# A convolution and two feed-forward layers on one core: the head of the kernel rebuilt

## The reference, cut to what matters

```python
# x: (2, 4096, 192), weight_gen: (2, 4096, 8, 7), all fp32
w = exp(weight_gen - max(weight_gen, -1)); w = w / (sum(w, -1) + 1e-9)       # softmax over the 7 taps
a[s, head, :] = sum_k w[s, head, k] * x_padded[s + k, head, :]               # 8 heads of 24 columns
h = maximum(a @ w_in1, 0); b = (h * h) @ w_out1                              # 192 -> 2048 -> 192
g = b @ w_in2;             out = (g * cos(g)) @ w_out2                       # 192 -> 2048 -> 192
```

## Time and profile before

| | us |
|---|---|
| median of three runs | 1240.97 |
| lowest, highest | 1236.84, 1241.13 |
| the profiled execution | 1241.01 |
| its span | 1239.2 |
| PE busy | 1192.4 (96%) |
| DVE busy | 976.0 (79%) |
| ACT busy | 813.8 (66%) |
| POOL busy | 369.4 (30%) |

### The profile page before, as it was taken

One profiled execution on the slowest core, in us unless ns is written; L12 is line 12 of the kernel. 1 busy time (PEld: TensorE's weight loads), 2 busy tenths in 40 slices (PEclk: granted clock), 3 DMA queues, 4 the chain that ended last, 5 costly groups with the idle time before them and its releaser, 6 DMA issues.

```text
span 1239.2 us, 24972 instructions
## 1 busy us (share of the span) xinstructions
PE 1192.4 (96%) x9571; PEld 1104.4 (89%) x9571; DVE 976.0 (79%) x1497; ACT 813.8 (66%) x1471; POOL 369.4 (30%) x245
## 2 busy tenths in 40 slices
PE   2888999999999999999999999999999999999997
PEld 1555879999999999999999999999999999999986
DVE  6775768787887878788787878778787878878786
ACT  1468666676666667676666667666666666666665
POOL 3734833426133060604315070422507051000000
PEclk9887999999999999999999999999999999999999
DMA  6440101111111110011111011111111010100000
GB/s 130 108 102 20 35 12 38 21 42 19 34 26 33 27 33 12 16 37 24 33 27 33 14 27 25 22 33 27 33 24 36 9 19 2 27 2 14 1 14 14
DMA packets 112918, 37.27 MB, mean 30 GB/s; under 512 B 101536, under 2 KB 110752, under 8 KB 112800
## 3 DMA queue, kind: packets, MB, share of 16 engines
q1 hardware_dynamic: 111488, 35.19, 13.9%
q10 hardware_dynamic: 1312, 0.49, 0.2%
HBM read 23.84 MB, written 6.29 MB: 24 GB/s over the span
## 4 chain that ended last, share of the span: by engine, by line
PE 94%; DVE 3%; ACT 1%; issue 1%; DMA 1%; SPq 0%; DVEq 0%; ACTq 0%
PE y L508 46%; PE h L508 43%; PE y L537 1%; PE h L525 1%; DVE x L1037 1%; DMA xc<-in_x_dram 1%; PE h L526 0%; PE h L527 0%; PE y L538 0%; PE y L542 0%; PE y L541 0%; PE y L540 0%; DVE g_lo L1084 0%; DVE h L1047 0%; DVE gen L955 0%
## 5 line engine op out<-in xcount | busy, mean ns | idle before, releaser
L508 PE MATMUL y<-g_hi,wo 64*128 64x512 f32 x2916 | 651.7, 394 | 0.0
L508 PE MATMUL y<-g_lo,wo 64*128 64x512 f32 x1944 | 494.2, 391 | 0.0
L508 PEld LDWEIGHTS y<-g_hi,wo 64*128 64x128 f32 x2916 | 401.5, 184 | 23.4 <-DVE xa_lo L1076 2.8
L466 POOL TENSOR_TENSOR tap<-xc,gen 128x768 f32<-128x768 f32 x105 | 162.1, 1550 | 593.3 <-DVE xd_lo L1059 579.1
L508 PEld LDWEIGHTS y<-g_lo,wo 64*128 64x128 f32 x1944 | 296.1, 184 | 5.8
L863 ACT ACTIVATE turns<-turns 128x512 f32<-128x512 f32 x239 | 151.0, 632 | 190.2 <-DVE turns L1051 189.2
L1070 DVE TENSOR_TENSOR h<-h,turns 128x512 f32<-128x512 f32 x239 | 166.5, 697 | 123.3 <-ACT turns L863 122.4
L508 PE MATMUL h<-xa_hi,wa_hi 64*128 64x512 f32 x974 | 257.3, 398 | 2.5 <-DVE xd_lo L1059 1.9
L508 PE MATMUL h<-xa_hi,wa_lo 64*128 64x512 f32 x974 | 253.7, 392 | 0.0
L508 PE MATMUL h<-xa_lo,wa_hi 64*128 64x512 f32 x974 | 253.1, 392 | 0.0
L1047 DVE SCALAR_TENSOR_TENSOR h<-h,relu 128x512 f32<-128x512 f32 x256 | 178.4, 697 | 84.2 <-ACT relu L836 81.3
(11 more groups left out here) (98 smaller groups left out, 1201.6 us busy)
## 6 DMA issues: line engine op xcount, KB each, us to landing
xc<-in_x_dram SPq DMA_DIRECT2D x62, 240.0 KB
out_dram<-arena SPq DMA_DIRECT2D x64, 64.0 KB, 1.9
xt_a<-x_blocks SPq DMA_DIRECT2D x224, 16.0 KB, 1.8
arena<-in_moe_w_out_dram SPq DMA_DIRECT2D x16, 192.0 KB, 2.8
arena<-in_moe_w_in_dram SPq DMA_DIRECT2D x16, 128.0 KB, 2.4
out_dram<-arena SPq DMA_DIRECT2D x60, 32.0 KB, 1.7
xt_d<-x_blocks SPq DMA_DIRECT2D x112, 16.0 KB, 1.8
gen<-in_weight_gen_dram SPq DMA_DIRECT2D x4, 392.0 KB, 8.6
```

The source lines that it names most:

```text
L466: pool.tensor_tensor(tap[:, k % 2, :].rearrange("p (r g) -> p r g", g=GROUP), rows[k], wk, ALU.mult).then_inc(pool_step, 1)
L508: return pe.matmul(o, w[rows, :], x[rows, :], start=start, stop=stop)
```

## The change

- `piece_lo` for VectorE and GpSimd are two functions now. VectorE does pieces 0 (its input part), 2, 4 to 7, and 8, 9, 10 (`scalar_tensor_tensor` from the unscaled piece), GpSimd the output part of 0, and 1, 3 and 11 to 15. VectorE's are spread over two slots each. ScalarE scales while it writes the high part, and scales in place only for GpSimd's pieces of layer two.
- GpSimd does nothing while VectorE convolves tile 0.
- Softmax in nine parts of 4, 4, 8, 8, ... token rows; from part 2 on GpSimd subtracts the maximum (`shift`). Reduce max of parts 2 to 8 behind slots 3 to 9, the later steps where a tile needs them.
- The first slot waits for each operand in turn, not for all of them.
- From step 2 to 18 a slot is a `head_slot`: its ups and downs are halves on alternating rows. Steps 19 and 20 use the paired form without the downs of layer two.
- Tile 1 is turned behind slot 11, into y2 (tile 0: one half into y2, one into y1), which the second layer uses only from step 21. Its split is in slot 12. Tile 2 is turned at slot 6 and split at slot 11 of tile 1 (before: 10 and 15).
- The loads of the first x rows are dealt anew: quarters 0 and 1 on SyncE, 2 and 3 on ScalarE.

```diff
     def turn_at(t):
-        return (SLOTS - 3, SLOTS - 6, SLOTS // 2 - 2)[t] if t <= PEEL else TURN
+        return (SLOTS - 5, SLOTS - 10)[t] if t < PEEL else TURN
     def split_at(t):
-        return (SLOTS - 3, SLOTS - 1, SLOTS // 2 + 3)[t] if t <= PEEL else SPLIT
+        return (SLOTS - 4, SLOTS - 5)[t] if t < PEEL else SPLIT
...
-        WARM_UP = 16
-        HI_AFTER = {(0, 0): (2,), (0, 2): (3,), (0, 4): (4,), (0, 6): (5,), (0, 8): (6,), (0, 10): (7,),
-                    (0, 11): (8,), (0, 12): (9,), (0, 13): (10,), (0, 14): (11,),
-                    (1, 0): (12,), (1, 1): (13,), (1, 2): (14,), (1, 3): (15,)}
-        LO_AFTER = {(0, 1): (2,), (0, 3): (3,), (0, 5): (4,), (0, 7): (5,), (0, 9): (6,), (0, 11): (7,)}
-        POOL_PIECES = range(PL, PIECES)
-        PARTS = [0, 2 * JJ, 6 * JJ, 11 * JJ, OWN]
-        SOFTMAX_AFTER = {(0, 2): [(1, 0)], (0, 3): [(1, 1)], (0, 6): [(1, 2), (1, 3)],
-                         (0, 8): [(2, 0)], (0, 10): [(2, 1)], (0, 12): [(3, 0)], (0, 13): [(3, 1)],
-                         (1, 0): [(2, 2), (2, 3)], (1, 1): [(3, 2), (3, 3)]}
-        EXPS_AFTER = {(0, 4): (1,), (0, 15): (2, 3)}
+        WARM_UP = 12
+        HI_AT = {4: 2, 5: 4, 6: 6, 7: 8, 8: 9, 9: 11, 10: 13, 11: 14, 12: 16, 13: 18, 14: 22, 15: 25}
+        for pc, n in HI_AT.items():
+            for op in range(3):
+                HI_AFTER.setdefault(n + op * (n > SLOTS), []).append((pc, op))
+        LO_AT = {2: 2, 4: 4, 5: 6, 6: 8, 7: 10, 8: 12, 9: 14, 10: 18}
+        POOL_LO = (3, 11, 12, 13, 14, 15)
+        for pc, n in LO_AT.items():
+            LO_AFTER.setdefault(n, []).extend([(pc, 0), (pc, 1)])
+            LO_AFTER.setdefault(n + 1, []).append((pc, 2))
+        PARTS = [0] + [JJ * t for t in range(1, TILES + 1) if t == 1 or t % 2 == 0]
+        LOADS = [0, 2, 5, len(PARTS) - 1]
+        SOFTMAX_AFTER = {0: [(1, 2), (1, 3)]}
+        SOFTMAX_AFTER.update({n: [(n - 1, 0)] for n in range(3, 10)})
+        SOFTMAX_AFTER.update({12: [(2, 2)], 13: [(2, 3)], 29: [(3, 2)], 30: [(3, 3)]})
+        SOFTMAX_AFTER.update({2 * SLOTS + 6 + k: [(4 + k // 2, 2 + k % 2)] for k in range(10)})
+        EXPS_AFTER = {n: n - 9 for n in range(11, 18)}
+        SIN_AFTER = 17
...
+            pool.wait_ge(piece_ready[0], 2)
+            for op in range(2):
+                piece_lo(1, op)
+            piece_lo(0, 2)
+            piece_lo(1, 2)
+            for op in range(3):
+                piece_lo(3, op)
+            scale(1)
+            pool.wait_ge(gen_scaled, 2)
             pool.wait_ge(x_loaded, FIRST_X + NEXT_X)
             convolve(1)
+            for part in range(2, len(PARTS) - 1):
+                shift(part)
+            scale(2)
+            pool.wait_ge(gen_scaled, 3)
             pool.wait_ge(x_loaded, FIRST_X + NEXT_X * 2)
             convolve(2)
+            for pc in POOL_LO[1:]:
+                for op in range(3):
+                    piece_lo(pc, op)
...
+            def head_slot(t, i, par, o, down):
+                n = SLOTS * t + i
+                fresh = i == D1 and t > 0
+                ups_of_slot(t, i, n, n - LAG)
+                if fresh:
+                    for k in range(3):
+                        up_a(o, 0, i, par, TOP, k, start=k == 0)
+                downs_of_slot(n, n - LAG)
+                y1_free(t, i, y1_summed)
...
+                for k in range(2):
+                    if not fresh:
+                        up_a(o, 0, i, par, TOP, k, start=k == 0)
+                    last = down_d(down, BOTTOM, k, start=k == 0)
+                last.then_inc(y1_d_left, 1)
+                if not fresh:
+                    up_a(o, 0, i, par, TOP, 2)
+                y1_free(t, i, y1_read)
...
+                for k in range(3):
+                    last = down_a(down, BOTTOM, k, start=k == 0)
+                    last_up = up_d(o, 0, i, par, k)
...
+                down_d(down, TOP, 0)
+                down_d(down, TOP, 1, stop=True).then_inc(y1_d_done, 1)
+                pe.wait_ge(y1_a_left, n - D1 + 1)
+                down_a(down, TOP, 0)
+                pe.wait_ge(h1_left, n - D1 + 1)
+                up_a(o, 0, i, par, BOTTOM, 0)
+                down_a(down, TOP, 1)
+                up_a(o, 0, i, par, BOTTOM, 1)
+                down_a(down, TOP, 2, stop=True).then_inc(down1_done, 1)
+                up_a(o, 0, i, par, BOTTOM, 2, stop=True).then_inc(up1_done, 1)
+                if (t, i) == (0, turn_at(0)):
+                    pe.wait_ge(x1_ready, 1)
+                    pe.wait_ge(x1_split, 2)
+                    for part in range(2):
+                        turn_x1(1, part)
...
+                last = act.activation(hi, w, ACT.Copy, scale=by)
+                if l and pc in POOL_LO:
+                    last = act.activation(w, w, ACT.Copy, scale=by)
```

More of the change, by code:

```diff
@@ L498, in _ @@
             for t in range(3, TILES):
+                if t % 2 == 0:
+                    scale(t // 2 + 1)
+                    pool.wait_ge(gen_scaled, t // 2 + 2)
                 pool.wait_ge(x_loaded, FIRST_X + NEXT_X * t)
@@ L555, in down_d, with turn_x1 @@
                             stop=stop and f == SLOTS - 1)
-            def turn_x1(i, part):
+            def turn_x1(t, part):
                 for jj in range(JJ):
                     at = jj * DM + part * DA
-                    for side, bank in enumerate(turn_banks(i)):
+                    for side in range(2):
                         rows = slice(side * DD, (side + 1) * DD)
-                        o = h[:, bank, part * TOK // 2:(part + 1) * TOK // 2].rearrange("p (q j n) -> p j q n", j=JJ, n=BLOCK)
+                        o = turn_banks(t, part)[:, side, part * TOK // 2:(part + 1) * TOK // 2].rearrange(
+                            "p (q j n) -> p j q n", j=JJ, n=BLOCK)
                         last = pe.transpose(o[:, jj], x1[rows, at:at + P], ident[rows, rows])
[L565 to L572, removed]
+                last.then_inc(x1_turned, 1)
             def ups_of_slot(t, i, n, m):
@@ L949, in softmax @@
                 if op == 0:
-                    dve.wait_ge(gen_loaded[min(part, 1)], 16 * QUARTERS)
+                    dve.wait_ge(gen_loaded[sum(part >= a for a in LOADS[1:])], 16 * QUARTERS)
                     dve.tensor_reduce(stat_view(part), gen_view(part), axis=AX.X,
@@ L1010, in tail_chunk, with piece_lo, low @@
                     turn_y2_d(TILES - 2)
+            def piece_lo(pc, op):
+                l, q = divmod(pc, PL)
+                r = pc % RING
+                cols = slice(q * PIECE, (q + 1) * PIECE)
+                fs = slice(q * PF, (q + 1) * PF)
+                rows = slice(l * DD, (l + 1) * DD)
+                by = [INV_2PI, 2.0 * math.pi] if l else [1.0, 1.0]
+                dve.wait_ge(piece_hi[pc], op + 1)
+                if op:
+                    dve.wait_ge(piece_ready[pc], op)
+                def low(o, w, hi, by):
+                    if l == 0:
+                        return dve.tensor_tensor(o, w, hi, ALU.subtract)
+                    return dve.scalar_tensor_tensor(o, w, by, hi, ALU.mult, ALU.subtract)
+                if op == 0:
+                    last = low(wa_lo[l][:, cols], stage_a[:, r, :], wa_hi[l][:, cols], by[0])
+                elif op == 1:
+                    last = low(wd_lo[rows, cols], stage_d[rows, r, :], wd_hi[rows, cols], by[0])
+                else:
+                    low(wo[l][:, fs, DM:2 * P], stage_o[:, r, :, DA:DM], wo[l][:, fs, DA:DM], by[1])
+                    last = low(wo[l][:, fs, 2 * P:2 * DM], stage_o[:, r, :, 0:DA], wo[l][:, fs, 0:DA], by[1])
+                last.then_inc(piece_ready[pc], 1)
             def convolve_first():
@@ L1091, in _ @@
             dve.memset(x1[:, JJ * DM:], 0.0).then_inc(pad_zeroed, 1)
-            for op in range(4):
+            for part in range(2):
+                for op in range(2):
+                    softmax(part, op)
+            for op in range(2, 4):
                 softmax(0, op)
```

323 lines of the change are left out of this document (157 added, 166 removed).

## The result

The changed kernel takes 1219.4 us (median of four runs, 1218.3 to 1220.5), the kernel before beside it 1239.9; the ratio is 0.984, 95% interval 0.982 to 0.986. 1218.0 us was forecast. The profiled execution took 1220.16 us against 1241.01: 20.9 us less.

A forecast was written before the change was run, and what follows sets the result against it. Only the head could move, with VectorE, made to wait beside GpSimd, setting much of its pace. Slot 22 starting 19.3 us earlier and 3.7 us from slot 32 took 1241.0 to 1218.0 us; range 1203 to 1231.

The forecast's parts named there:

- the walk: The prediction's slot-by-slot timing of the head from the start: slot 10 at 66.5 us, slot 18 at 91, slot 22 at 109.
- the three signs that I had named for being wrong: VectorE waiting for the convolution in slot 22, TensorE waiting for a piece's low part, or half clock past 40 us.
- First convolution: VectorE's start of the head: with GpSimd idle its 13 instructions take 12.0 us, ending at 23.7 us, 2.8 us earlier.
- Head slot of 2.6 us: TensorE from slot 2: halves on alternating rows take 2.6 us at full clock against 2.96, about 4.8 at half clock.
- the rival of 1222 us: TensorE's head slots: weight loads between same-row halves are exposed, costing 4.6 us in all; chance 0.04.
- VectorE bound, slots 3 to 9: VectorE, stretched beside GpSimd until 58.5 us, sets the time at 3.2 to 5.4 us a slot; slot 10 at 66.5.
- The price of these waits: Rival in the head: with piece work never waiting for GpSimd, slots 3 to 9 cost 2.9, not 4.3 us; chance 0.18.
- a case that stays low throughout: TensorE's clock: half-row matmuls don't bring it up, slots 2 to 18 take 4.8 us each, total 1256 us; chance 0.06.
- Slots 10 to 17: Late head: slot 10 starts at 66.5 us and slot 18 at 91, against 69.93 and 101.99 before.
- Slots 18 to 21: End of the head: slot 18 at 91 us, slot 22 at 109 instead of 128.27, three slots in 13.5 us.
- Slot 32: The stall waiting for tile 2's split goes, as tile 2 is turned and split earlier: 3.7 us gained.
- all behind it moves with it: After the head: everything behind slot 22 starts earlier by slot 22's 19.3 us, but for the stall at slot 32.

The follow-up runs named there:

- c0: The changed kernel itself, run again unchanged beside the next three runs: 1219.8 us, ratio 0.985 to the kernel before.
- a3: The changed kernel with GpSimd's low parts of pieces 1 and 3 done beside VectorE's first convolution: 1223.0 us, ratio 0.987 to the kernel before.
- a2: The changed kernel with slots 2 to 18 in the old 128-row form instead of halves: 1219.6 us, ratio 0.985 to the kernel before.
- a4: The changed kernel with VectorE's low parts reading one SBUF input, a one-element reduction that computes something else: 1208.0 us, ratio 0.976 to the kernel before.
- a1: The changed kernel with tile 2 turned behind slot 10 and split in slot 15 of tile 1, as before: 1225.6 us, ratio 0.990 to the kernel before.
- b2: The changed kernel with the sums of softmax parts 4 to 8 spread over tiles 2 to 6: 1217.9 us, ratio 0.984 to the kernel before.
- c3: The changed kernel minus halves, early tile 2, tile 1's new turning, GpSimd's silence in the first convolution and layer-two scaling change: 1230.9 us, ratio 0.994.

## Why the prediction was right

The time, its sign and the sum were right (23.0 us forecast, 20.9 measured), and so was the mechanism: VectorE late in the head, stretched beside GpSimd. That the sum came so near is partly luck, as its steps were off in both directions: the changed kernel was 5.5 us ahead of the walk at slot 10, 4.4 at slot 18 and 1.2 at slot 22. Two of the three signs that I had named for being wrong did show: TensorE waited for a piece's low part (wd_lo, 1.99 us ahead of slot 4), and half clock came back past 40 us (48.86 to 52.27, 59.10 to 62.51 and 89.8 to 93.2 us). The third, VectorE waiting for tile 2's convolution in slot 22, did not: that ended at 102.64 us and VectorE turned its result at 113.41.

- *First convolution*: expected end 23.7 us, measured 22.45. The x rows came at 10.9 us, not 11.7 (9.9 in c0's trace), and the 13 instructions took 11.6, not 12.0. a3 shows the cause: 3.3 us of the gain are GpSimd's silence. From the last sum to the first relu 3.95 us passed where I had 3.2 for the end of slot 0; before, it was 6.0.
- *Head slot of 2.6 us*: right at full clock; slots that wait for nothing are 2.57 us apart, so weight loads between halves on the same rows are not exposed and the rival of 1222 us falls. But the form brings nothing in a2. Where the clock does fall, it may help it up again, see the last section. At half clock the walk's 4.8 us don't follow from the rows that it names, whose ratio gives 2.6 x 2.86 / 1.40 = 5.3; the trace has halves 0.43 us apart, 11 of them 4.7 us.
- *VectorE bound, slots 3 to 9*: right in kind. I had slot 10 at 66.5 us; it started at 61.0. The convolution on GpSimd began 2.3 us before I had it and ended at 54.1, not 58.5, and the input part of a piece cost 2.4 to 3.0 us beside it, not 3.4: one of its two instructions was short each time (0.72, 0.99, 1.01 us), when GpSimd's instruction was nearly done.
- *The price of these waits*: 1203 us was given for none, a4 has 1208.0; the walk put 15 us on them, they are 11.7, with the falls of the clock that came with them and that the walk didn't have. The Trainium skill's rule ("SBUF — State Buffer", "Who interferes with whom"), that two SBUF inputs are what contends, agrees with a4, and with `scalar_tensor_tensor` in the rows above (0.41 us alone, 1.72 beside GpSimd), which the trace of before could not show.
- *The clock*: this I had only as a case that stays low throughout. It came up at 31.8 us and fell in four stretches beside waits of 2 us and less; a walk by VectorE's times alone doesn't have this. From relu to relu, slots 4, 7 and 9 took 5.4 to 6.3 us, their waits included.
- *Slots 10 to 17*: 24.5 us expected (66.5 to 91), 25.6 measured (61.0 to 86.6). That most of the gain lies from slot 10 on was in the walk: 3.4 us ahead at slot 10, 19.3 at slot 22.
- *Slots 18 to 21*: 18 us expected (91 to 109), 21.2 measured (86.6 to 107.8). The first three of them took 15.1 us, not 13.5. The clock was at 0.50 from 89.8 to 93.2 us, and the split of y1's d part, two SBUF inputs again, took 2.32 us.
- *Slot 32*: 3.7 us expected, 4.0 measured between the traces; undone by itself (a1) it is 6.
- *Slots 22 to 31*: "all behind it moves with it" was wrong by 2.1 us; the relus of slots 22 to 27 are 4.45 to 4.72 us apart and the chain of waits runs through VectorE and ScalarE; a1 puts 0.9 us on the early split, the rest wasn't divided. The ten sums in tile 2 cost another 1.5, which I had put at nothing; b2 gets them back. These two, 3.6 us, are the term that the sum lacked; the 1.2 us ahead at slot 22 and 0.3 more at slot 32 bring it to the 2.1 us by which the sum is off.

## What to carry to other kernels

Where GpSimd works long instructions beside VectorE, count VectorE's instructions with two inputs in SBUF, not its columns: here 0.41 us became up to 1.9, and the same number of columns through one input made the kernel 11.7 us faster. Here VectorE set the pace, and the shorter matmul form brought nothing. Look for stops behind which the clock is low: in slots 10 to 20 of the kernel before, two stops of 2.65 and 3.32 us stood ahead of 20 us at half clock, and the greater part of the gain was made where they had been. Work that is dealt out of a head to "later, where there is room" has to be put against the room in that very slot.

## What was not expected of the hardware

The granted clock fell to 1.2 GHz for 3.4 us beside waits of 1.65 to 2.01 us when slots were made of 64-row halves, in slots 3 to 9 three times in one trace and twice in another of the same kernel. The length of the wait alone doesn't decide it: in that second trace no fall came with a wait of 1.77 us ahead of slot 7, nor in a2 with one of 2.03 us ahead of slot 21. With 128-row matmuls (a2) it did not fall in slots 3 to 9, where the waits were 0.8 us at most, though it took until 41.8 us to come up (41.4 in the kernel before, 30.3 and 31.8 with halves).

How long it stayed low also differed. In slots with 128-row matmuls it was 10.2 us behind a wait of 1.75 us (c3), and 6.8 and 13.8 us behind 2.65 and 3.32 us (the kernel before); in slots of halves, with no second wait in the stretch, it was 3.4 us each time but once (6.7 us in a3, beside a wait of 3.3 us). No run changes the form alone behind the same wait, so that halves bring the clock back sooner is likely and not shown. With the waits filled by three matmuls a slot it stayed at 2.4 GHz from 30.1 to 81.3 us.
